# A convolution and two MLPs on one core: where the first tile is convolved, and how its taps reach the partitions

## The reference

```python
w = softmax(weight, axis=-1)                  # weight: 8 heads x 7 taps
x_pad = concatenate([zeros(B, 6, D), x])      # x: 2 x 4096 x 192, 24 channels a head
attn[b, s, c] = sum_k w[head(c), k] * x_pad[b, s + k, c]
h = attn.reshape(8192, 192) @ moe_w_in        # 192 x 2048
y = maximum(0.01 * h, h) @ moe_w_out          # 2048 x 192
h2 = y @ moe2_w_in                            # 192 x 2048
g2 = where(h2 >= 1, h2, where(h2 <= -1, 0, (h2 + 1)**2 / 4))
out = g2 @ moe2_w_out                         # 8192 x 192, float32
```

## Time and profile before

| | |
|---|---|
| three executions, median (lowest to highest) | 1160.63 us (1158.31 to 1160.77) |
| the profiled execution | 1160.67 us |
| its span, first to last instruction | 1158.9 us |
| mean granted TensorE clock | 0.999 |
| PE busy | 1152.2 us, 99%, 9746 matmuls |
| DVE, ACT, POOL busy | 896.0, 799.2, 50.9 us |

### The profile page before, as it was taken

The page is one execution under the profiler, slowest core; times in us unless marked ns, Lnnn a source line. Parts: engine busy times, 40 slices in busy tenths (PEclk is TensorE's granted clock), DMA queues, the critical chain, the costliest instruction groups (busy, mean ns, idle before and its releaser), DMA issues.

```text
span 1158.9 us, 25672 instructions
## 1 busy us (share of the span) xinstructions
PE 1152.2 (99%) x9746; PEld 926.0 (80%) x9746; DVE 896.0 (77%) x1509; ACT 799.2 (69%) x1474; POOL 50.9 (4%) x76
## 2 busy tenths in 40 slices
PE   9999999999999999999999999999999999999998
PEld 6788888888888888888888888888888888888886
DVE  7787877787777887778877777777787877878665
ACT  6768667585775857758577685766758567685685
POOL 5533000000000000000000000000000000000000
PEclk9999999999999999999999999999999999999999
DMA  5330100101001010010100101000010100100001
GB/s 139 95 78 2 18 12 1 29 2 26 4 1 29 1 28 1 1 29 1 28 1 10 20 1 29 1 15 16 1 29 1 25 5 1 29 1 15 1 1 28
DMA packets 114440, 21.95 MB, mean 19 GB/s; under 512 B 106128, under 2 KB 114320, under 8 KB 114320
## 3 DMA queue, kind: packets, MB, share of 16 engines
q1 hardware_dynamic: 112144, 19.68, 9.3%
q10 hardware_dynamic: 2176, 0.66, 0.3%
HBM read 14.02 MB, written 6.29 MB: 18 GB/s over the span
## 4 chain that ended last, share of the span: by engine, by line
PE 97%; DVE 1%; ACT 1%; issue 0%
PE hidden L417 15%; PE hidden L415 10%; PE hidden L411 10%; PE hidden L413 10%; PE acc_edge L475 10%; PE acc_main L481 10%; PE acc_main L483 10%; PE acc_main L485 10%; PE acc_edge L472 10%; PE hidden L627 1%; DVE g_lo L929 0%; DVE g L918 0%; PE hidden L613 0%; ACT pre L667 0%; PE acc_main L511 0%
## 5 line engine op out<-in xcount | busy, mean ns | idle before, releaser
L686 ACT CAST g_hi<-g 128x512 fp32r<-128x512 f32 x510 | 299.2, 619 | 294.6 <-PE acc_main L513 245.5
L929 DVE TENSOR_TENSOR g_lo<-g,g_hi 128x512 fp32r<-128x512 f32 x510 | 335.2, 691 | 121.2 <-ACT g_hi L686 116.7
L417 PE MATMUL hidden<-op_edge,w_edge 64*128 64x512 f32 x768 | 260.6, 393 | 0.0
L923 DVE SCALAR_TENSOR_TENSOR g<-hidden,pre 128x512 f32<-128x512 f32 x256 | 176.7, 690 | 107.4 <-ACT pre L674 104.5
L411 PE MATMUL hidden<-op_hi,w_main 64*128 64x512 f32 x512 | 201.2, 393 | 0.3 <-DVE g L918 0.3
L429 PE MATMUL hidden<-op_hi,w_main 64*128 64x512 f32 x512 | 201.3, 393 | 0.0
L433 PE MATMUL hidden<-op_hi,w_main 64*128 64x512 f32 x512 | 201.2, 393 | 0.0
L413 PE MATMUL hidden<-op_lo,w_main 64*128 64x512 f32 x512 | 201.1, 393 | 0.0
L438 PE MATMUL hidden<-op_edge,w_edge 64*128 64x512 f32 x512 | 201.0, 393 | 0.0
L415 PE MATMUL hidden<-op_hi,w_main 64*128 64x512 f32 x512 | 201.0, 392 | 0.0
L431 PE MATMUL hidden<-op_lo,w_main 64*128 64x512 f32 x512 | 201.0, 392 | 0.0
(11 more groups left out here) (126 smaller groups left out, 2790.2 us busy)
## 6 DMA issues: line engine op xcount, KB each, us to landing
x_in<-in_x_dram SPq DMA_DIRECT2D x67, 64.0 KB, 2.2
out_dram<-y_main SPq DMA_DIRECT2D x62, 64.0 KB, 1.9
stage<-in_moe_w_out_dram SPq DMA_DIRECT2D x15, 192.0 KB, 2.7
x_in_edge<-in_x_dram SPq DMA_DIRECT2D x68, 32.0 KB, 1.9
out_dram<-y_edge SPq DMA_DIRECT2D x32, 64.0 KB, 1.8
stage<-in_moe_w_in_dram SPq DMA_DIRECT2D x15, 128.0 KB, 2.4
stage<-in_moe_w_in_dram SPq DMA_DIRECT2D x30, 64.0 KB, 2.4
stage<-in_moe_w_out_dram ACTq DMA_DIRECT2D x1, 192.0 KB, 3.4
```

Source lines behind the costliest of these rows:

```text
L417: done = nc.tensor.matmul(h[:], w_edge[l][top, i - 3, cols], op_edge[l][b][top, :], start=i == first, stop=False)
L686: nc.scalar.copy(hi_of(n, c)[:], g[c % SLOTS][:]).then_inc(g_hi_ready, 1)
L929: nc.vector.tensor_tensor(lo_of(n, c)[:], g[c % SLOTS][:], hi_of(n, c)[:].bitcast(F32), ALU.subtract).then_inc(g_lo_ready, 1)
```

## The change

The taps' DMA broadcasts all 56 weights to each of the 128 partitions. The softmax runs there on 128 partitions x 8 heads, and a mask `own` from POOL (head by partition, for main and edge) picks each partition's own taps by a multiplication and a sum on DVE. The spreading matmuls, `head_of` and the two ACT copies go. The conv of tile 0 is divided: columns 0 to 383 of the main part are seven taps on DVE into acc_main[0], and columns 384 to 511 are seven matmuls on PE into acc_edge[1], with diagonals made by POOL. The edge conv is seven matmuls of 256 columns on PE into acc_edge[0], with diagonals made by ACT. `keep_warm(8)` becomes `keep_warm(16)`, `keep_warm(2)` goes, and the opening begins with the main products. ACT starts two of the four loads of x_in_edge. DVE transposes tile 1 and computes its first four taps behind all of tile 0.

```diff
-WARM = 8
-WARM_ON = 2
+WARM = 16
+SPLIT = 3 * T // 4
...
+        main_diag = [pre[i // 4][:, (i % 4) * P:(i % 4 + 1) * P] for i in range(TAPS)]
+        edge_diag = [g[1 + i // 4][:, (i % 4) * P:(i % 4 + 1) * P] for i in range(TAPS)]
+        first_part, last_part = slice(0, SPLIT), slice(SPLIT, T)
+        first_main = acc_main[0][:, first_part]
+        last_main = acc_edge[1][:, 0:T - SPLIT]
+        first_edge = acc_edge[0][:, 0:HALF]
...
             load_x_main(EVEN, 0, parts=P // Q - 1)
-            load_x_edge(EVEN, 0)
+            load_x_edge(EVEN, 0, parts=range(2))
             load_weights(1)
...
+            pool.wait_ge(same_step, 3)
+            pool.wait_ge(taps_ready, 1)
+            for i in range(TAPS):
+                nc.gpsimd.tensor_scalar(main_diag[i], same, taps[:, 0, i:i + 1], None, ALU.mult
+                                        ).then_inc(main_diag_ready, 1)
...
-                for c, i in (0, 3), (0, 4), (1, 3), (0, 0), (0, 2), (1, 0), (0, 1):
-                    top_first(job, c, i, first=3)
+                for i in (0, 2, 1, 3, 4):
+                    top_first(job, 0, i)
                 for i in range(2):
-                    top_first(job, 1, 2 - i, first=3)
+                    top_first(job, 1, i)
+                for i in range(2):
+                    top_first(job, 1, i + 2)
                     bottom_first(job, 0, i)
...
             keep_warm(WARM)
-            pe.wait_ge(head_of_ready, 1)
-            pe.wait_ge(taps_step, 6)
-            for a in (0, 1):
-                nc.tensor.matmul((acc_main, acc_edge)[a][0][:, 0:TAPS], head_of[:, a, :], taps_head[:],
-                                 start=True, stop=True).then_inc(taps_spread, 1)
-
-            keep_warm(WARM_ON)
             pe.wait_ge(x_turned, 1)
             for i in range(TAPS):
-                pe.wait_ge(diag_ready, i + 1)
-                last = nc.tensor.matmul(hidden[3][:], diag[i], x_main[0][:, i:i + T], start=i == 0, stop=i == TAPS - 1)
-            last.then_inc(main_convolved, 1)
+                pe.wait_ge(main_diag_ready, i + 1)
+                last = nc.tensor.matmul(last_main, main_diag[i], x_main[0][:, SPLIT + i:T + i],
+                                        start=i == 0, stop=i == TAPS - 1)
+            last.then_inc(last_convolved, 1)
+            pe.wait_ge(half_moved, 1)
+            for i in range(TAPS):
+                pe.wait_ge(edge_diag_ready, i + 1)
+                last = nc.tensor.matmul(first_edge, edge_diag[i], x_edge[0][:, i:i + HALF],
+                                        start=i == 0, stop=i == TAPS - 1)
+            last.then_inc(edge_convolved, 1)
...
-            act.dma_start(taps_raw[:], weight).then_inc(taps_loaded, 16)
+            act.dma_start(taps_raw[:], weight.partition_broadcast(P)).then_inc(taps_loaded, 16)
...
+            for q in (2, 3):
+                act.dma_start(x_in_edge[EVEN][Q * q:Q * (q + 1), :].rearrange("r (g c) -> r g c", c=Q),
+                              x_rows[:, GROUPS // 2:GROUPS, P + Q * (q % 2):P + Q * (q % 2) + Q]
+                              ).then_inc(x_edge_loaded[EVEN], 16)
...
-            act.wait_ge(taps_spread, 1)
-            nc.scalar.copy(taps[:, 0, :], acc_main[0][:, 0:TAPS]).then_inc(taps_ready, 1)
...
             for i in range(TAPS):
-                nc.scalar.activation(diag[i], same, ACT.Copy, scale=taps[:, 0, i:i + 1]).then_inc(diag_ready, 1)
-                if i == 0:
-                    act.wait_ge(taps_spread, 2)
-                    nc.scalar.copy(taps[:, 1, :], acc_edge[0][:, 0:TAPS]).then_inc(taps_ready, 1)
-                if i == 2:
+                nc.scalar.activation(edge_diag[i], same, ACT.Copy, scale=taps[:, 1, i:i + 1]).then_inc(edge_diag_ready, 1)
+                if i == 4:
                     move_half((0, EVEN, 0))
+            last_hi()
             round_weights(0)
             round_weights(1)
+            first_hi()
             edge_hi((0, EVEN, 0))
-            main_hi((0, EVEN, 0))
-            edge_hi_low((0, EVEN, 0))
+            edge_low((0, EVEN, 0))
             edge_top((0, EVEN, 0))
             round_weights(2)
...
-            nc.vector.tensor_scalar(taps_sub[:], taps_raw[:], taps_max[:], None, ALU.subtract).then_inc(taps_step, 1)
+            nc.vector.tensor_tensor(taps_sub[:], taps_raw[:], taps_max[:].unsqueeze(2).to_broadcast([P, H, TAPS]),
+                                    ALU.subtract).then_inc(taps_step, 1)
...
-            nc.vector.tensor_scalar(taps_head[:], taps_exp[:], taps_inv[:], None, ALU.mult).then_inc(taps_step, 1)
+            nc.vector.tensor_tensor(own_inv[:], own[:, 0:2, :], taps_inv[:].unsqueeze(1).to_broadcast([P, 2, H]),
+                                    ALU.mult).then_inc(taps_step, 1)
+            nc.vector.tensor_tensor(own_taps[:], taps_exp[:].unsqueeze(1).to_broadcast([P, 2, H, TAPS]),
+                                    own_inv[:].unsqueeze(3).to_broadcast([P, 2, H, TAPS]),
+                                    ALU.mult).then_inc(taps_step, 1)
+            nc.vector.reduce_sum(taps[:], own_taps[:].rearrange("p s h i -> p s i h"), AX_X).then_inc(taps_ready, 1)
             turn_x_main(first)
+            dve.wait_ge(taps_ready, 1)
+            first_tap(0)
             turn_x_edge(first)
-            dve.wait_ge(taps_ready, 2)
-            for i in range(TAPS):
-                edge_tap(first, i)
+            for i in range(1, TAPS):
+                first_tap(i)
+            last_lo()
+            first_lo()
+            edge_lo_first(first)
+            edge_lo_second(first)
             turn_x_main(second)
-            edge_lo_first(first)
-            main_tap(second, 0)
-            main_lo(first).then_inc(first_main_ready, 1)
-            edge_lo_second(first)
-            for i in (1, 2, 3):
+            for i in range(4):
                 main_tap(second, i)
```

More of the change, by code:

```diff
@@ L239, in bass_conv_mlp_mlp @@
         same = g[3][:, 0:P]
-        diag = [g[1 + i // 4][:, (i % 4) * P:(i % 4 + 1) * P] for i in range(TAPS)]
-        def main_of(t):
-            if is_number(t, 0):
-                return hidden[3]
-            return conv_main
+        main_diag = [pre[i // 4][:, (i % 4) * P:(i % 4 + 1) * P] for i in range(TAPS)]
[4 more added lines that the diff above has]
+        first_edge = acc_edge[0][:, 0:HALF]
         def main_sum(t, i):
@@ L280, in load_x_main, with load_x_edge @@
                                  x_rows[:, bass.ds(group, GROUPS), Q * q:Q * (q + 1)]).then_inc(x_loaded[b], 16)
-            def load_x_edge(b, pos):
+            def load_x_edge(b, pos, parts=range(P // Q)):
                 group = b * (S // Q) + pos * GROUPS
-                for q in range(P // Q):
+                for q in parts:
                     h, d = q // 2, P + Q * (q % 2)
@@ L387, in l_piece, with top_first @@
                 return PIECES * (n // 2) + c // PC
-            def top_first(job, c, i, first=0):
+            def top_first(job, c, i):
                 n, l, t, b = job["n"], job["layer"], job["t"], job["b"]
@@ L394, in top_first @@
                 h = hidden[c % SLOTS]
-                last = 1 if first else 4 - c % 2
+                last = 4 - c % 2
                 done = None
-                if i == first and is_number(n, 0, 2) and c % PC == 0:
-                    pe.wait_ge(weights_ready, l_piece(n, c) + 1)
-                if first and c == 0:
-                    if i == first:
-                        pe.wait_ge(edge_hi_ready, 2)
+                if is_number(n, 0) and c == 0:
                     if i == 0:
                         pe.wait_ge(main_rounded, 1)
+                        pe.wait_ge(weights_hi, 1)
                     if i == 1:
                         pe.wait_ge(first_main_ready, 1)
+                    if i == 2:
+                        pe.wait_ge(weights_ready, 1)
+                    if i == 3:
+                        pe.wait_ge(edge_hi_ready, 2)
+                if i == 0 and is_number(n, 0, 2) and c % PC == 0 and (n or c):
+                    pe.wait_ge(weights_ready, l_piece(n, c) + 1)
                 if i == 0:
@@ L410, in top_first @@
                         pe.wait_ge(g_ready, k - SLOTS + 1)
-                    nc.tensor.matmul(h[:], w_main[l][top, 0, cols], op_hi[l][b][top, :], start=first == 0, stop=False)
+                    nc.tensor.matmul(h[:], w_main[l][top, 0, cols], op_hi[l][b][top, :], start=True, stop=False)
                 elif i == 1:
-                    done = nc.tensor.matmul(h[:], w_main[l][top, 0, cols], op_lo[l][b][top, :], start=False, stop=False)
+                    nc.tensor.matmul(h[:], w_main[l][top, 0, cols], op_lo[l][b][top, :], start=False, stop=False)
                 elif i == 2:
@@ L417, in top_first @@
                     done = nc.tensor.matmul(h[:], w_edge[l][top, i - 3, cols], op_edge[l][b][top, :],
-                                            start=i == first, stop=False)
+                                            start=False, stop=False)
```

(22 more changed lines are left out.)

107 lines of the change are left out of this document (62 added, 45 removed).

## The result

| | before | after |
|---|---|---|
| median of the executions (lowest to highest) | 1160.54 us (1158.31 to 1160.77) | 1140.78 us (1140.65 to 1160.97) |
| ratio, after to before | | 0.9834, interval 0.9814 to 0.9853 |
| the profiled execution, its span | 1160.67, 1158.9 us | 1140.85, 1139.1 us |
| mean granted TensorE clock | 0.999 | 0.998 |
| first activation (DVE's g of chunk 0) | 18.98 us | 19.67 us |

The kernel is 19.8 us faster, where 1.2 was forecast, and outside the range. The one execution of after at 1160.97 us had no like when the kernel was timed again (five executions in e1); no run explains it, and nothing rests on it.

The account below looks back on a forecast made before the run. PE's steady part was taken as full and untouched, the end as set by a DVE and ACT chain from the first activation. That activation at 17.75 instead of 18.98 us gave 1160.67 - 1.23 = 1159.4 us, range 1157.6 to 1162.0.

Parts of the forecast that it names:

- step 1: Taps at the start: two more ACT loads, six DVE steps taking 1.5 us; ready at 5.55 us, before 5.63.
- rival D: Broadcast taps or x_in land later under two added loads; lateness above 1.1 us counts once; 1160.7 us; chance 0.12.
- Step 4: PE's start: warm-up ends 7.35, POOL's diagonals (0.37 each) 8.15, main conv 9.0, edge conv 12.0, readable by ACT 12.2 us.
- Steps 2 and 3: SyncE's remaining loads about 1 us earlier, worth nothing; DVE's seven taps of tile 0, 0.65 us each, end at 11.3.
- Step 5: ACT's casts: weight casts done at 11.4, first 384 columns at 11.9, three edge casts at 13.45 us.
- Step 6: DVE's backlog after the edge conv: subtraction, transpose of tile 1, four taps; first activation at 17.75 instead of 18.98 us.
- a first g that moves while the later PE waits do not: Listed sign that the forecast is wrong; rightly, first g near 17.8 and the g_lo wait near 44.8 us.
- A: Rival: PE's start, not DVE's backlog, sets the end; first pair's 2.8 us gain is kept, 1157.9 us; chance 0.08.
- C: Rival: clock stays low through the edge conv, edge passes 0.43 us; activation 4.8 us late, 1165.4 us; chance 0.07.
- B: Rival: clock's rise moment varies; before 1158.7 us if up from start, after 1158.9 to 1160.8; ends outside own case 0.08.
- the early end of B: Clock up at 4.9 us and quick taps: conv ends 11.65, first activation 17.2, kernel 1158.9 us; counted toward faster.

Follow-up runs that it names:

- e1: The kernel after, unchanged, timed again in five rounds: 1140.65 us against 1159.02 for the kernel before, ratio 0.9838.
- e5: The kernel before with 128 B a partition of unused SBUF in front of x_in, giving later tensors their addresses in after: 1138.75 us, ratio 0.9815.
- e6: The kernel after with `own` and `taps_den` allocated last, so x_in and what follows lie where before had them: 1161.35 us, ratio 1.0016.
- e12: The kernel after with POOL making four of the seven main diagonals and ACT the last three: 1139.65 us, ratio 0.9828.
- e13: The kernel before with 64 unused bytes ahead of the weights, so weights and operands both lie 64 bytes higher: 1159.39 us, ratio 0.9999.
- e10: The kernel before with 256 unused bytes a partition ahead of x_in, moving its operands: 1159.04 us, ratio 0.9997.
- e15: The kernel before with 96 unused bytes a partition ahead of x_in, moving its operands: 1159.02 us, ratio 0.9997.
- e4: The kernel before with the longer warm-up alone, keep_warm(16) in place of keep_warm(8): 1160.34 us, ratio 1.0007.
- e7: The kernel before with the opening of the kernel after (`top_first` and `opening`) alone: 1161.05 us, ratio 1.0011.
- e3: The kernel before with five idle DVE memsets ahead of its jobs, to make a PE gap and a clock drop: 1163.62 us, ratio 1.0034.
- e8: The kernel before with 192 unused bytes a partition ahead of x_in, moving its operands: 1158.82 us (1153.72 to 1159.94), ratio 0.9983.
- e16: The kernel after with SyncE's x loads held back until the taps have landed: 1140.49 us, ratio 0.9835.
- e17: The kernel after with 192 unused bytes ahead of x_in, bringing weights and operands to distance 0: 1129.97 us, ratio 0.9743.

## Why the prediction was wrong

**The step that failed** is the first one, on what bounds the kernel: "so that part has no room, and the change adds nothing to it and takes nothing from it". The row said that PE was never idle. It did not say that a pass has one fixed cost. What the runs showed in its place: PE's spacing depends on where its operands lie, and the diff moved them, by resizing tensors that have nothing to do with the steady part. That alone is worth 20 us (e5 without the change, 1138.75 us; e6 with the change and without the move, 1161.35). None of the rivals held this; step 1 counted the instructions on the resized tensors and not their bytes. 4850 pairs by 4.4 ns outweigh everything else in the text.

**The change's own sum** had the wrong sign too: +0.69 us on the first activation (18.98 to 19.67) in place of -1.23. That the whole came out faster, as forecast, has nothing to do with it. By its steps:

- Step 1, mis-sized. The load of 128 rows landed 1.76 us later than that of 8 (3.97 against 2.21), and 1.1 were taken as covered. Taps were ready at 6.31, not 5.55. The six DVE steps took 1.56 us (4.75 to 6.31), as taken (1.5). This is a part of rival D, 0.76 us of it. Even the covered part isn't free: the wait for the taps also holds up ACT's loads of weight piece 0, by 1.8 us.
- Step 4, mis-sized. A POOL diagonal is 4.09/7 = 0.58 us, outside the bounds of 0.29 to 0.44, which came from other operations. Seven of them end at 10.59, not 8.15, and PE waits for each. The main conv ends at 11.1, not 9.0. The clock was better than taken, up at 3.95 us in this trace with the warm-up over at 6.28 in place of 7.35, and it didn't help, since POOL was last. The edge conv took 3.04 us for 3.0, but ends at 14.2, not 12.2. e12 shows POOL's part by taking some of it away.
- Steps 2 and 3 held: six DVE taps at 0.65 (3.88/6), hidden.
- Step 5, wrong but hidden. It starts the weight casts at 9.3 and has the cast of 384 columns over at 11.9. In after that cast ends at 13.86, and in e12, with POOL's part reduced, at 13.24, because weight piece 0 lands only at 10.69. POOL repaired, this would have kept the edge casts at about 13.2, as in e12, in place of 12.2.
- Step 6 held: the first activation comes 5.5 us behind the edge conv, for 5.55 forecast. PE's gap of about 2 us is there, 1.8, ended by DVE. The claim that the first activation sets the end, one for one, is borne out by e12.
- The check "a first g that moves while the later PE waits do not" can't be read in after, where PE lost its lead in the low clock, but it can in other traces, and the waits move with the first g. In before that is at 18.98 us and the wait for g_lo ends at 46.02. In e12 they are at 18.64 and 45.52, in e1 at 19.68 and 46.54:

```profile
46.54 0.50 PE L488 MATMUL acc_edge<-g_lo,w_out 64*128 64x512 f32 x1 [0.24 <-DVE g_lo L982]
```

```profile
45.52 0.49 PE L489 MATMUL acc_edge<-g_lo,w_out 64*128 64x512 f32 x1 [0.24 <-DVE g_lo L988]
```

**The rivals.** A did not happen: the first pair came earlier than before (15.80 against 16.73) and the change still costs time. C did not: the 14 edge passes took 0.22 each. D happened in part, as said. B's mechanism was seen. The granted clock of kernels that start as before does rises at different moments, at 10.42 us in the trace of before and 5.51 in e13's, in which the conv of tile 0 took 6.25 us where it had taken 7.97:

```profile
6.27 6.25 PE L628 MATMUL hidden<-x_main,g 128*128 128x512 f32 x14
...
12.56 0.59 ACT L718 CAST op_hi<-hidden 128x512 fp32r<-128x512 f32 x1 [0.22 <-PE hidden L628]
```

That execution took 1158.39 us. This bears out what the Trainium skill, "TensorE: Matmul & The Clock Gate", Part 1, says of a run-variable moment of the rise, which no run showed at the time of the prediction. It fits the times of before, which in e1's rounds fall into two groups, nine at 1158.4 to 1159.1 us and seven at 1160.1 to 1160.9. e13's execution belongs to the first; before's (1160.67), e10's (rise at 10.35, 1160.63) and e15's (9.87, 1160.42) belong to the second. It also fits that the change costs 2 us by the medians and less between late traces: e6 comes 0.70 us later than before to its first activation and took 1161.14 against 1160.67. In the seven traces of after's start the rise ranges from 3.95 to 7.11 us, and the first activation stays at 19.56 to 19.69 (18.64 in e12), since PE's warm-up isn't last there; so the moment is absorbed, as B said, but at a level that is later than both of before's. That the long warm-up by itself narrows the range is not shown: e4 has it and ranges over 1.5 us, e7 has the short one and ranges over 0.6.

**The chances.** The 0.15 for faster counted the early end of B, but that end, 1158.9, lies above the 1158.3 that it was to reach; only A's 0.08 did.

**Open:** why the distance between weights and operands matters. No view shows reads of SBUF. The five distances follow no simple order (-64 is nearly as good as 0, -32 is not). Distances of less than 32 B, and each kind of weights against its own operand, were not tried, and -64, -32 and 128 only with the weights at 128. That only addresses mod 256 count rests on e10, one shift by 256 B.

## What to carry to other kernels

A PE that reads 100% busy at full clock can still get faster: count its passes in a fixed window, or take the spacing of their starts, before writing that a part is untouched. Any edit that resizes or adds a tensor moves the ones behind it, so compare an edit with a version whose other tensors stay put (an unused tensor does that), and try a few paddings of 64 B by themselves; here one was worth 32 us, and the change under study by itself cost 2. Cost an engine's operation by a row of that very operation on that engine: near ones on POOL, 0.29 and 0.44 us for what took 0.58, were too low by a quarter to a half. And ask what else stands behind a late wait on the same engine: here it was the loads of the weights.

## What the hardware showed that was not expected

- Pairs of 64-row fp32r passes of 512 columns start every 226.7, 228.9 or 233.3 ns, by (weights' address less operand's address) mod 256 of 0, -64, or 64 and -32; at 128 it is 233.0. For the same instructions that is 1128, 1139 and 1159 us.
- The busy time of the weight loads goes from 160 to 199 us of 200 at the same spacing of 233.3 ns (e6, e3), by how far the two row halves are out of step. At the distance 128 (e8) the executions scatter over 6 us.
- A partition-broadcast load of 56 values to 128 partitions was in use 3.2 us after its issue (0.79 to 3.97), one of 8 rows 1.8 us sooner, and still 1.6 us sooner than the broadcast with SyncE's loads held back (e16).
- POOL's multiplication of a 128x128 fp32 tile by a scalar per partition takes 0.58 us, its selection 0.29.
- PE standing still for 1.8 us from 18.7 us on was followed by a clock of 0.50 from 21.0 to 24.4 us in the traces of after and (from 20.8) of e17, and by none in those of e1 and e6. It cost nothing (1140.85 with, 1140.86 without), since PE was not what the end waited for.
